# Transposes of the attention probabilities moved behind the whole down product, in a one-core attention and two-stage MoE kernel

## What is computed

```
p_packed = sm_attn(p, k, v)            # 32 packed queries per head over 576 keys
x = sm_attn(q, p_packed, p_packed)     # each token over the 32 packed rows
h = x @ w_in                           # 512 -> 1024
solu = h * softmax(h);  ln = layernorm(solu) * g_ln
x = ln @ w_out                         # 1024 -> 512
e = argmax(x @ w_gate);  out = prob_e * (relu(x @ w1[e]) @ w2[e])
```

## Time and profile before

| what | value |
|---|---|
| runs | 1098.42, 1098.95, 1099.76 us (median 1098.95) |
| profiled execution: time, span | 1097.72 us, 1096.1 us |
| PE busy | 1012.6 us (92%) |
| DVE busy | 505.2 us (46%) |
| ACT busy | 447.8 us (41%) |
| POOL busy | 284.9 us (26%) |
| mean busy share of the 16 DMA engines between 200 and 500 us | 0.23 to 0.28 |
| granted clock of PE, mean of the execution | 0.966 |

### The profile page before, as it was taken

The page is one execution under the profiler, slowest core; times in us unless marked ns, Lnnn a source line. Parts: engine busy times, 40 slices in busy tenths (PEclk is TensorE's granted clock), DMA queues, the critical chain, the costliest instruction groups (busy, mean ns, idle before and its releaser), DMA issues.

```text
span 1096.1 us, 20129 instructions
## 1 busy us (share of the span) xinstructions
PE 1012.6 (92%) x5707; PEld 795.5 (73%) x5708; DVE 505.2 (46%) x1219; ACT 447.8 (41%) x767; POOL 284.9 (26%) x637
## 2 busy tenths in 40 slices
PE   7548999999999999999994999999999999999994
PEld 4336777777777777777873788888888888888883
DVE  3344666565666656576565252521152431234211
ACT  2344555555555555566552241421241322233110
POOL 1421222222222222245562121221121221222211
PEclk9758999999999999999997999999999999999998
DMA  9301222322122221151103551511152331111110
GB/s 354 108 11 51 67 66 78 97 87 88 58 61 85 87 79 38 37 195 50 39 20 116 193 191 48 190 40 48 38 170 69 114 125 38 46 40 38 48 38 29
DMA packets 64759, 92.62 MB, mean 84 GB/s; under 512 B 42944, under 2 KB 45120, under 8 KB 64704
## 3 DMA queue, kind: packets, MB, share of 16 engines
q1 hardware_dynamic: 55584, 61.96, 17.8%
q0 software_dynamic: 9120, 29.97, 8.0%
HBM read 70.37 MB, written 21.54 MB: 84 GB/s over the span
## 4 chain that ended last, share of the span: by engine, by line
PE 89%; DVE 3%; issue 2%; ACT 2%; DMA 1%; POOL 1%; SPq 0%; ACTq 0%; POOLq 0%; DVEq 0%
PE ps L1341 39%; PE ps L1428 12%; PE ps L1348 8%; PE ps L1407 7%; PE ps L1435 6%; PE ps L1416 3%; PE ps L1377 3%; PE ps L1306 2%; PE ps L1455 2%; PE ps L1263 2%; PE ps L1283 2%; DVE m_odd L915 1%; PE ps L1272 1%; PE ps L1219 1%; POOL w_in L440 1%
## 5 line engine op out<-in xcount | busy, mean ns | idle before, releaser
L1341 PE MATMUL ps<-W,xr 128*128 (+1 forms) x912 | 224.4, 401 | 2.4 <-DVE xr L1084 2.4
L1341 PE MATMUL ps<-W,zr 128*128 x912 | 222.2, 398 | 2.6 <-DVE zr L1157 2.6
L1341 PEld LDWEIGHTS ps<-W,xr 128*128 128x128 f32 x912 | 170.0, 190 | 41.7 <-DVE xr L1084 1.8
L1341 PEld LDWEIGHTS ps<-W,zr 128*128 128x128 f32 x912 | 168.3, 188 | 41.0 <-issue 2.8
L1428 PE MATMUL ps<-w_out,zr 128*128 128x512 f32 x576 | 156.8, 410 | 1.1 <-ACT zr L721 1.1
L1428 PEld LDWEIGHTS ps<-w_out,zr 128*128 128x128 f32 x576 | 101.9, 188 | 39.5 <-issue 16.9
L802 ACT ACTIVATE zr<-ps 128x1024 fp32r<-128x1024 f32 x38 | 39.0, 1025 | 196.6 <-PE ps L1348 196.6
L457 POOL TENSOR_TENSOR small<-half 128x1 f32<-128x1 f32 x77 | 21.6, 280 | 345.1 <-DVE yb L1169 195.4
L461 POOL TENSOR_TENSOR sbuf<-sbuf,msum 128x256 f32<-128x256 f32 x36 | 22.2, 616 | 283.0 <-DVE msum L978 283.0
L797 ACT ACTIVATE hbuf<-ps 128x1024 f32<-128x1024 f32 x38 | 38.8, 1022 | 137.6 <-PE ps L1341 137.6
L1084 DVE TENSOR_TENSOR xr<-ps,xr 128x512 fp32r<-128x512 f32 x39 | 26.9, 691 | 145.6 <-ACT xr L792 145.6
(11 more groups left out here) (216 smaller groups left out, 1486.5 us busy)
## 6 DMA issues: line engine op xcount, KB each, us to landing
raw_e<-w_exp SPq DMA_DIRECT2D x48, 512.0 KB, 5.0
qb<-y_sorted POOLq DMA_DIRECT2D x40, 257.0 KB, 3.0
vb<-v_t SPq DMA_DIRECT2D x16, 640.0 KB, 5.6
kb<-k_t SPq DMA_DIRECT2D x16, 576.0 KB, 4.4
qb<-q_t SPq DMA_DIRECT2D x144, 64.0 KB, 3.0
y_sorted<-pad SPq DMA_DIRECT2D x8, 257.0 KB, 4.2
raw_out<-w_moe SPq DMA_DIRECT2D x4, 512.0 KB, 5.0
raw_in<-w_moe SPq DMA_DIRECT2D x4, 512.0 KB, 14.3
```

The source lines that it names most:

```text
L1341: mm = nc.tensor.matmul(dst, lhs[:, a, k * P:(k + 1) * P], rhs(b, cols), start=(first and n == 0), stop=(last and n == 2))
```

## The change

In PE's loop the call of `turn_a(t + 1)` is moved. It stood between the first three and the last five chunks of the low down product, ahead of the second half of the unit's weights (`m_half(v, 1)`) and of `k_pack(u)`. It now stands behind all of these, directly ahead of `turn_z(t)`. Nothing else is changed; the lists of ACT and DVE stay word for word as they were.

```diff
                 if there(t - 1):
                     down_lo(t - 1, range(0, 3))
-                if there(t + 1):
-                    turn_a(t + 1)
                 if v is not None:
                     m_half(v, 1)
                 if u is not None:
                     k_pack(u)
                 if there(t - 1):
                     down_lo(t - 1, range(3, KF))
+                if there(t + 1):
+                    turn_a(t + 1)
                 if there(t):
                     turn_z(t)
```

## The result

The changed kernel takes 1115.96 us (median of 4 runs, 1114.26 to 1118.39), the kernel before 1098.68 us (1098.12 to 1099.76); the ratio is 1.0158, 95% interval [1.0137, 1.0179]. It is slower, by 17.3 us. The forecast was 1117 us.

A forecast was written before the change was run, and what follows sets the result against it. PE bounds the kernel, holding 89% of the chain of waits. Terms 9.9 + 3.8 + 0.8 + 1.8 + 1.6 = 17.9 us on 1097.72 give 1115.6; with 1.2 for the runs' median, 1117 us, range 1107 to 1124 (78%).

The forecast's parts named there:

- The wait in a v turn: 12 v turns: PE restarts at `m_half(v, 1)` 0.22 us earlier, still stopped by `m_lo(v, 0)`; PE gains 0.13 us a turn.
- v turn into u turn: 9 times: late `a_hi` delays ACT's list, `k_et` and `k_pack` by 0.85 us; with 0.26 for transposes, 1.1 each, 9.9 us.
- The cover: u turns: transposes formerly done while PE would have waited for `k_et` now come on top, 0.26 us ahead of `turn_z`.
- v turn into plain turn: 3 times, m = 8 into m = 0: the 1.4 us shift reaches `copy_lt` and delays `turn_logits`; 1.25 each, 3.8 us.
- The sign that I had named: Plain turns behind v turns: L1461 would wait for L732 over 1 us three times.
- u turn behind plain turn: 3 times, m = 1: ACT comes in time, only the transposes' lost cover counts; 0.26 each, 0.8 us.
- Late v turn: 3 times, m = 7 into 8: `k_pp`, behind `a_lo` on DVE, comes late for `k_turn_pp`; 0.6 each, 1.8 us.
- Last group: Plain turns t = 27 to 34: later `turn_a` and `first_hi` on ACT delay `copy_lt`; 0.2 each, 8 turns, 1.6 us.
- the wait goes: Rival: the wait at `turn_a` vanishes and nothing replaces it; 16.0 us less, 1083 us; chance 2%.
- lateness is absorbed: Rival: ACT's lateness is absorbed but the transposes' cover in u turns is lost; 3.4 us, 1102 us; chance 7%.
- it runs on into the next v turn: Rival: late `a_hi` of a u turn also delays the next `m_hi(v, 0)`, 0.7 in 12 turns; 26 us, 1125 us; 9%.

The follow-up runs named there:

- the split wait: Changed kernel, but in a group's first turn only the up product's second half waits for the last `m_lo(v, 1)`, the first half for the one before; one run, 1110.56 us.
- the v turns alone: Kernel before, with the transposes directly behind `m_half(v, 1)` in v turns and at their old place in all others; 1097.12 us, ratio 0.9976.
- the place ahead of the five chunks: Kernel before, with the transposes behind `m_half(v, 1)` and `k_pack` but ahead of the last five chunks of the down product; 1099.44 us, ratio 1.0004.
- the first experiment: Kernel before, with the transposes at their old place in u turns and at the new one in all others; 1117.51 us, ratio 1.0157.
- the combined kernel: Kernel before, with the change plus `m_half(v, 0)` moved ahead of the down product's fourth to sixth high chunks; 1108.03 us, ratio 1.0082.

## Why the prediction was right, step by step

- **The wait in a v turn.** Right: the stop moved to L1306 and shrank only by the 0.22 us between the ends of L915 and L1025. Forecast 0.13 a turn, measured 0.19.
- **v turn into u turn.** The mechanism is shown from both sides: undoing ACT's lateness alone takes u turns from +9.5 to +1.9, making it alone gives +6.3. Forecast 1.1 us for the two turns together, measured 0.83 to 0.95, so 7.8 us in place of 9.9. Counted from the end of `m_lo(v, 0)`, `m_hi(v, 1)` moved by 1.5 (1.6 forecast), `squares` by 1.3 (1.4), `k_et` by 0.6 (0.85), `k_pack` by 0.6. The term was too large at the last link: `k_et` starts 1.15 us behind `squares` where I had put 1.25, and each earlier shift was 0.1 too long. The cover was worth 0.22 in place of 0.26: `turn_a` adds 0.34 ahead of the load of `turn_z`, but that load then runs 0.13 less ahead of its matmuls.
- **v turn into plain turn.** The place was wrong, and that the amount came near is luck. I had priced `copy_lt` and `turn_logits` (1.25 us). The first wait is that of the up product in the first turn of a group for the last `m_lo(v, 1)` (L1400), which I had overlooked: in the kernel before that subtraction ended at 344.41, 0.07 ahead of the load of L1407 at 344.48, with hardly any slack (the rows stand below). It costs 1.65 us. The sign that I had named, L1461 behind L732 over 1 us three times more, didn't come: PE's stops there (3, 2.6 us, 0.9 the longest) are the same in both kernels. The term I named stands right behind it, as the split wait showed, and takes back over half of the 0.85 us expected to be saved there. The rows of the kernel before:

```profile
343.02 1.39 DVE L915 TENSOR_TENSOR m_even<-ps,m_even 64x512 fp32r<-64x512 f32 x2 [1.16 <-ACT m_even L650]
...
344.48 1.70 PEld L1407 LDWEIGHTS ps<-m_even,aTr 128*128 128x128 f32 x8
```

- **u turn behind plain turn.** Forecast 0.26, measured 0.21.
- **Late v turn.** Forecast 0.6 for `k_pp`; measured 0.35 + 0.19 = 0.54, since the gain of a v turn is inside.
- **Last group.** Forecast 8 x 0.2 = 1.6; measured 2.0, of which 0.6 in t = 35, where no scores stand ahead of the up product, and 0.0 in t = 31.
- **Sum.** 17.9 us forecast; 16.2 by these turns, 17.3 by the medians. Against these turns the u term was 2.1 too high and the late v turns 0.8 (their own gain was not in the sum) and the u turns behind plain turns 0.4 (t = 1 isn't counted here); the plain turns were 1.2 too low and the last group 0.4. They partly cancelled, so the sum came closer than its parts, which is luck.
- **Rivals.** That the wait goes was excluded twice (the change itself; the v turns alone). That lateness is absorbed is true only in u turns and up to about 0.5 us (the place ahead of the five chunks), not at 1.6; a plain turn behind a v turn paid 0.48 even there. That it runs on into the next v turn didn't happen: all v turns but the late one got shorter.

What stays open is the clock in the first experiment and in one turn of the combined kernel.

## What to carry to other kernels

When an instruction waits, look at what the next one in the list waits for before moving the first behind it; here both waited for the same subtraction, 0.22 us apart. Then follow what the moved instruction releases: on an engine with an in-order list, everything queued behind its reader is moved too, and the price is the smallest slack further down, not the idle share of that engine. To remove a repeated stop, move the producer of what is waited for (here 11 us by the turns, 12.5 by the medians, for three matmuls moved ahead of six), not the waiter.

## What the runs showed of the hardware beside this

The granted clock can differ behind equal stops of PE (1.56 us in both kernels above), and half clock for some 3 us then cost 1.6 us, as much again as the stop.

A small DVE instruction beside a long POOL one: in the last group of the changed kernel L1047 was late enough to fall into POOL's `first_lo` (L509), and it ended only with it.

```profile
513.77 2.40 POOL L509 TENSOR_TENSOR W<-raw_e,W 128x1024 fp32r<-128x1024 f32 x1 [2.76 <-ACT W L753]
...
514.77 1.42 DVE L1047 SCALAR_TENSOR_TENSOR rk_hot<-rk,hot 128x8 f32<-128x8 f32 x1
...
516.42 1.23 DVE L1019 TENSOR_TENSOR zr<-zraw,zr 128x1024 fp32r<-128x1024 f32 x1 [0.22 <-ACT zraw L727]
...
516.58 1.12 POOL L473 TENSOR_SCALAR small<-small 128x1 f32<-128x1 f32 x1
```

L1047 took 1.42 us where it takes 0.17 in the v and u turns. In the kernel before it met only the end of L509 (488.30, 0.22 us). It cost nothing here: `z_lo` waited for ACT until 516.42 anyway. The reverse stands in the same rows: POOL's L473, 0.19 us elsewhere, took 1.12 and ended within 0.1 us of the long L1019 beside it (times on POOL are rough).
